# A two-layer Strassen kernel on one core: x of two tiles gets a second home and later splits, and ScalarE copies one PSUM partial sum in more phases

## The reference

```python
x = attention(q, k, v, mem_k, mem_v)              # 3072 x 512
h = x @ moe_w_in                                  # 512 -> 2048
g = np.where(h > 0.0, h, np.exp(np.minimum(h, 0.0)) - 1.0)
x = g @ moe_w_out                                 # 2048 -> 512
r = np.maximum(x @ moe2_w_in, 0.0)
out = (s * (r * r) + b) @ moe2_w_out
```

## Time and profile before

| what | value |
|---|---|
| median of 3 runs | 1153.65 us (1152.37 to 1153.94) |
| profiled execution: its own time | 1152.69 us |
| its span, first to last instruction | 1151.0 us |
| busy share: PE, DVE, ACT, POOL | 96%, 73%, 67%, 34% |
| mean share of the 16 DMA engines' time on the main queue | 84.9% |

### The profile page before, as it was taken

One profiled execution on the slowest core, in us unless ns is written; L12 is line 12 of the kernel. 1 busy time (PEld: TensorE's weight loads), 2 busy tenths in 40 slices (PEclk: granted clock), 3 DMA queues, 4 the chain that ended last, 5 costly groups with the idle time before them and its releaser, 6 DMA issues.

```text
span 1151.0 us, 18156 instructions
## 1 busy us (share of the span) xinstructions
PE 1100.9 (96%) x5787; PEld 876.8 (76%) x5787; DVE 843.8 (73%) x1258; ACT 767.7 (67%) x1806; POOL 392.1 (34%) x427
## 2 busy tenths in 40 slices
PE   7989988989899999989999999999999999999998
PEld 4767666767677777768788787887888888888886
DVE  4895787368957956896887968868848569576485
ACT  4886786577657757756758667667666366674564
POOL 5788789751231432234276113653000000000000
PEclk8998999989999999999999999999999999999999
DMA  9998999999799889859899789998697666776664
GB/s 210 258 272 260 348 321 354 347 286 327 212 269 249 259 244 272 274 184 329 306 357 343 242 260 376 298 351 273 194 275 233 189 198 186 216 220 190 195 189 158
DMA packets 204055, 302.81 MB, mean 263 GB/s; under 512 B 112824, under 2 KB 121016, under 8 KB 203960
## 3 DMA queue, kind: packets, MB, share of 16 engines
q1 hardware_dynamic: 203960, 301.65, 84.9%
HBM read 226.10 MB, written 75.50 MB: 262 GB/s over the span
## 4 chain that ended last, share of the span: by engine, by line
PE 68%; DMA 7%; ACT 6%; POOL 6%; DVE 5%; issue 4%; SPq 4%; ACTq 0%; POOLq 0%; DVEq 0%
PE ps L1003 33%; PE ps L988 30%; DMA w_scratch<-w_new 4%; POOL w_new L786 2%; ACT ps L1083 2%; DMA w_ring<-w_scratch 1%; POOL att L786 1%; ACT elu L1169 1%; PE ps L900 1%; DVE g_lo L1464 1%; SPq L592 1%; PE ps L925 1%; ACT elu L1174 1%; PE ps L952 1%; DVE X L1381 1%
## 5 line engine op out<-in xcount | busy, mean ns | idle before, releaser
L988 PE MATMUL ps<-xc_hi,w_ring 128*128 128x512 f32 x1344 | 435.4, 397 | 6.1 <-DVE X L1433 3.1
L1003 PE MATMUL ps<-g_hi,w_ring 128*128 128x512 f32 x1344 | 421.7, 395 | 15.9 <-issue 7.6
L1003 PEld LDWEIGHTS ps<-g_hi,w_ring 128*128 128x128 f32 x1344 | 249.6, 189 | 75.4 <-issue 14.9
L988 PEld LDWEIGHTS ps<-xc_hi,w_ring 128*128 128x128 f32 x1344 | 253.9, 189 | 64.1 <-issue 3.2
L988 PE MATMUL ps<-xc_lo,w_ring 128*128 128x512 f32 x672 | 263.2, 392 | 0.0
L1003 PE MATMUL ps<-g_lo,w_ring 128*128 128x512 f32 x672 | 263.2, 392 | 0.0
L786 POOL TENSOR_TENSOR w_new<-w_raw,w_new 128x256 fp32r<-128x256 f32 x179 | 165.8, 932 | 226.7 <-ACT w_new L1222 223.8
L1464 DVE TENSOR_TENSOR g_lo<-X,g_hi 128x512 fp32r<-128x512 f32 x240 | 176.9, 741 | 26.1 <-ACT g_hi L1208 25.4
L1208 ACT ACTIVATE g_hi<-X 128x512 fp32r<-128x512 f32 x240 | 148.8, 627 | 62.2 <-PE ps L1003 59.8
L1381 DVE TENSOR_TENSOR X<-s,ps 128x512 f32<-128x512 f32 x144 | 96.1, 682 | 104.6 <-ACT s L1145 77.1
L1003 PEld LDWEIGHTS ps<-g_lo,w_ring 128*128 128x128 f32 x672 | 126.9, 189 | 27.0
(11 more groups left out here) (117 smaller groups left out, 1339.2 us busy)
## 6 DMA issues: line engine op xcount, KB each, us to landing
w_ring<-w_scratch SPq DMA_DIRECT2D x336, 512.0 KB, 4.4
w_scratch<-w_new SPq DMA_DIRECT2D x179, 256.0 KB, 5.3
w_scratch<-att SPq DMA_DIRECT2D x45, 256.0 KB, 5.3
w_raw<-in_moe_w_in SPq DMA_DIRECT2D x16, 512.0 KB, 6.2
w_raw<-in_moe_w_out SPq DMA_DIRECT2D x16, 512.0 KB, 6.2
x_scratch<-y SPq DMA_DIRECT2D x12, 512.0 KB, 6.2
att<-x_scratch SPq DMA_DIRECT2D x12, 512.0 KB, 6.3
out<-elu SPq DMA_DIRECT2D x24, 256.0 KB, 4.4
```

Of the source, the lines that this page charges most:

```text
L988: last = nc.tensor.matmul(bank_of(st.pi, st.i), w[:, a, cols], x[:, st.pi, kk, :], start=(st.pi in (P1, P5, P4) and kk == 0 and n == 0), s ...
L1003: last = nc.tensor.matmul(bank_of(st.pi, d), w[:, a, cols], x[:, k % RING, :], start=(st.pi in (P1, P5) + (P4,) * (1 - st.gr) and st.i == ...
```

## The change

One half of x of tiles 1 and 2 keeps its home in `elu`, the other (kk 1) gets the block X11 of X, which is free late in a down phase; the sums for P6 and P4 go to t_more. Both halves are loaded earlier than the first split (88 and 94), the splits stand at 102 to 105 and 110 to 119, and GpSimd makes three sums of each half and then one more of each. ScalarE copies U2 in every phase.

```diff
-SPLIT_AT = ((92, 93, 95, 96, 97, 98, 100), (107, 108, 110, 111, 113, 115, 117))
-LOAD_AT = (88, 102)
+SPLIT_AT = ((P1, 0, 102), (P1, 1, 103), (P2, 0, 104), (P2, 1, 105), (P5, 0, 110), (P5, 1, 111), (P6, 0, 112), (P6, 1, 113),
+            (P7, 0, 114), (P3, 0, 115), (P4, 0, 116), (P7, 1, 117), (P3, 1, 118), (P4, 1, 119))
+LOAD_AT = (88, 94)
...
-        x_raw = elu[:, :, :]
+        x_raw = [elu[:, :, :], X[:, X11, :, :]]
...
+            if t < TPL and pi in (P6, P4):
+                return t_more[:, kk, :]
             if t < TPL:
-                return x_raw[:, RAW_OF[pi], :]
+                return x_raw[kk][:, RAW_OF[pi], :]
...
-                    sp.wait_ge(x_lo_done, x_count(t) + 7 * kk)
-                    to = x_raw
+                    else:
+                        sp.wait_ge(g_lo_done, PHASE * (2 * t - 1) + QUADS * P5 + QUADS)
+                        sp.wait_ge(t_done, sums_done(t - 1, 1, P6, QUADS - 1))
+                    sp.wait_ge(x_lo_done, x_count(t))
+                    to = x_raw[kk]
...
-                nc.gpsimd.tensor_tensor(t1, x12, x11, ALU.subtract).then_inc(x_sums, 1)
...
+            def sums_of_x(t):
+                n = HEAD_SUMS + 8 * (t - 1)
+                for kk in range(2):
...
+                    pool.wait_ge(x_lo_done, x_count(t) + x_index(t, kk, P1) + 1)
+                    nc.gpsimd.tensor_tensor(x11, x12, x11, ALU.subtract).then_inc(x_sums, 1)
+                    pool.wait_ge(x_sums, n + 3 * kk + 1)
+                    nc.gpsimd.tensor_tensor(t2, x22, x11, ALU.subtract).then_inc(x_sums, 1)
+                    nc.gpsimd.tensor_tensor(x12, x22, x12, ALU.subtract).then_inc(x_sums, 1)
+                for kk in range(2):
+                    x21, t2 = x_from(t, kk, P2), x_from(t, kk, P6)
+                    pool.wait_ge(x_lo_done, x_count(t) + x_index(t, kk, P6) + 1)
+                    nc.gpsimd.tensor_tensor(t2, x21, t2, ALU.subtract).then_inc(x_sums, 1)
...
-                    if r % 6 == 5:
-                        pe.wait_ge(y12_u2, 2 * st.t + i + 1)
-                    else:
-                        pe.wait_ge(s2_done, copies_before(r) + i + 1)
+                    pe.wait_ge(s2_done, 2 * r + i + 1)
...
-                    act.wait_ge(x_lo_done, x_count(d.t + 1))
+                    act.wait_ge(x_lo_done, x_relu(d.t))
...
-                        if x == 12 + d and p.gr == 0:
+                        if x == 12 + d:
                             copy_s2(p.round, d, p.start + QUADS * P6 + 3)
...
-                dve.wait_ge(step_done, p.start + QUADS * P6 + 4)
+                dve.wait_ge(s2_done, 2 * p.round + d + 1)
                 dve.wait_ge(c12_done, 2 * (p.round - 3) + d + 1)
-                add(y_at(X12, d), y_at(X12, d), acc_e[d][:, :], y12_u2)
+                add(y_at(X12, d), y_at(X12, d), s2[:, d, :], y12_u2)
```

More of the change, by code:

```diff
@@ L163, in splits_at @@
     return made
-def copies_before(r):
-    return 2 * (r - r // 6)
 ITEMS0 = 8 * 4 * TPL
@@ L230 @@
 HEAD_ORDER = [(c, pi) for c, pi, _ in HEAD_SPLITS]
-SPLIT_AT = ((92, 93, 95, 96, 97, 98, 100), (107, 108, 110, 111, 113, 115, 117))
-LOAD_AT = (88, 102)
+SPLIT_AT = ((P1, 0, 102), (P1, 1, 103), (P2, 0, 104), (P2, 1, 105), (P5, 0, 110), (P5, 1, 111), (P6, 0, 112), (P6, 1, 113),
+            (P7, 0, 114), (P3, 0, 115), (P4, 0, 116), (P7, 1, 117), (P3, 1, 118), (P4, 1, 119))
+SPLITS = [(pi, kk) for pi, kk, _ in SPLIT_AT]
+LOAD_AT = (88, 94)
 SPLIT_LATE = ((P1, 0, 99), (P1, 1, 100)) + tuple((pi, kk, 106 + 2 * i + kk) for i, pi in enumerate((P2, P5, P6, P7, P4, P3))
@@ L260, in x_index @@
 def x_index(t, kk, pi):
-    return LATE.index((pi, kk)) if t >= TPL else 7 * kk + SPLIT_X.index(pi)
+    return (LATE if t >= TPL else SPLITS).index((pi, kk))
 def x_split_at(g):
[L265 to L272, removed]
+    return [(xt, kk, pi) for xt in range(1, TILES) for pi, kk, at in (SPLIT_AT if xt < TPL else SPLIT_LATE)
+            if g == PER_TILE * (xt - 1) + at]
 def out_block_at(g):
@@ L537, in late_sum, with x_relu, x_sum @@
             return 8 * (t - TPL) + 2 * (SUM_T[pi] - 1) + kk + 1
+        def x_relu(t):
+            return x_count(t) + x_index(t, 0, P4) + 1
+        def x_sum(t, kk, pi):
+            first = HEAD_SUMS + 8 * (t - 1)
+            return first + (7 + kk if pi == P4 else 3 * kk + {P5: 1, P6: 2, P7: 3}[pi])
         def sums_done(t, gr, pi, j):
@@ L807, in prepare @@
                     split_w(m, P3)
[L809 to L814, removed]
-                nc.gpsimd.tensor_tensor(t1, x12, x11, ALU.subtract).then_inc(x_sums, 1)
-                pool.wait_ge(x_sums, n + 1)
-                nc.gpsimd.tensor_tensor(x12, x22, x12, ALU.subtract).then_inc(x_sums, 1)
-                pool.wait_ge(x_lo_done, x_count(t) + x_index(t, kk, P3) + 1)
-                pool.wait_ge(x_sums, n + 2)
-                nc.gpsimd.tensor_tensor(t2, x22, t1, ALU.subtract).then_inc(x_sums, 1)
-                pool.wait_ge(x_lo_done, x_count(t) + x_index(t, kk, P2) + 1)
-                pool.wait_ge(x_sums, n + 3)
-                nc.gpsimd.tensor_tensor(t4, x21, t2, ALU.subtract).then_inc(x_sums, 1)
+            def sums_of_x(t):
+                n = HEAD_SUMS + 8 * (t - 1)
+                for kk in range(2):
+                    pool.wait_ge(x_in[kk], 32 * t)
+                    x12, x22 = (x_from(t, kk, pi) for pi in (P7, P3))
+                    x11 = x_from(t, kk, P1)
+                    t2 = x_from(t, kk, P6)
+                    pool.wait_ge(x_lo_done, x_count(t) + x_index(t, kk, P1) + 1)
[7 more added lines that the diff above has]
+                    nc.gpsimd.tensor_tensor(t2, x21, t2, ALU.subtract).then_inc(x_sums, 1)
             def sums_of_head(c):
@@ L847, in _ @@
             prepare(sets_of(PAIR))
-            for kk in range(2):
-                sums_of_x(1, kk)
+            sums_of_x(1)
             for m in range(SETS, SETS + 4):
                 prepare((m,))
-            for kk in range(2):
-                sums_of_x(2, kk)
+            sums_of_x(2)
             for m in range(SETS + 4, 2 * SETS):
```

5 lines of the change are left out of this document (2 added, 3 removed).

## The result

The change makes the kernel faster, by less than forecast. Eight runs of it have a median of 1150.19 us (1148.11 to 1152.94), eight of the kernel before 1153.8 us (1151.96 to 1155.89): a ratio of 0.997, with a 95% interval of 0.9955 to 0.9984. The forecast was 1147.8, 5.9 us under before; measured are 3.6.

A forecast was written before the change was run, and what follows sets the result against it. TensorE was taken to bound the kernel. The terms −7.6 + 3.0 (tile 1) and −4.1 + 2.8 (tile 0) gave −5.9, so 1153.65 became 1147.8 us; the range was 1141.5 to 1152.5, the forecast's own 1145.0 to 1150.5.

The forecast's parts named there:

- The loss removed: Where the next tile's x is prepared, all waits go: 7.6 us in tile 1, 4.1 in tile 0, together 11.7.
- The mechanism of the new waits: Six GpSimd sums hold the shared SBUF port, so a low part costs VectorE 1.65 us for 0.60; TensorE waits.
- +3.0 (tile 1): Last down phase of tile 1: new waits of 1.1 us at step 108 and 1.9 at step 109.
- +2.8 (tile 0): Tile 0: new waits of 1.5 us at step 108 and 1.0 to 1.1 at step 3 of tile 1; 2.7 to 2.8.
- the list: Timetable of VectorE's operations beside six sums, from step 102 in tile 1 and 103 in tile 0, giving each step's lateness.
- the window of 52 us: Expected profile window of tile 0's last down phase after the change; it was 53.19 before.
- Cost nothing, as said: Loads at 88 and 94, splits at 110 to 119 and ScalarE's U2 copies were each taken as 0 us.
- A: The sums cost nothing on TensorE's path, so all 11.7 us stay gained: 1142.0 us; chance 0.15.
- B: All nine low parts from step 104 on wait for the port, 6.4 us more: 1154.2 us; chance 0.12.
- C: The new waits lower the clock again, 1.7 us in each of tiles 0 and 1: 1151.2 us; chance 0.08.
- D: Weight loads collide with x at steps 100 to 104 of tiles 0 and 1, 9.4 us: 1157.2; chance 0.05.

The follow-up runs named there:

- narrow_sums: The changed kernel with GpSimd's sums of x for tiles 1 and 2 cut to 8 of 512 columns; 1143.14 us, 0.991 of before.
- before_narrow: The kernel before with its sums of x cut to 8 of 512 columns; 1146.67 us, 0.9937 of before.
- hold_half: The changed kernel with GpSimd's three sums of the second half of x held until step 111's low part is made; 1147.03 us, 0.9923 of before.
- late_p2: The changed kernel with the splits for P2 at 108 and 109 instead of 104 and 105; 1146.48 us, 0.9929 of before.
- u2_only: The kernel before with only ScalarE's copies of U2 in the last down phases; 1154.39 us, 1.0009 of before.
- x_only: The changed kernel without ScalarE's extra copies of U2; 1150.95 us, 0.9968 of before.
- spread_no_u2: The changed kernel, second-half sums held until step 111's low part, P2's splits behind P6's, without ScalarE's extra U2 copies; 1142.21 us, 0.9917 of before.
- spread: The changed kernel with the second half's sums held until step 111's low part and P2's splits behind P6's; 1143.87 us, 0.9901 of before.

## Why the prediction was right and wrong

**The loss removed: right.** The forecast was 11.7 us at two places; narrow_sums, which has everything of the change but the length of the sums, measures 11.5. The unit of steps 94 to 105 came to 20.70, and steps 96 to 103 of tile 1 have no wait but 0.14. How the 11.7 came about I had described, but not apportioned: 7.6 were the sums already (before_narrow, with the clock), the late load and the low parts of x in the queue the smaller part.

**The mechanism of the new waits: right.** Low parts at 1.74 to 1.78 us beside six sums, adds to y at 0.68, TensorE waiting at steps 108 and 109. narrow_sums shows the sums as the cause, hold_half and late_p2 that it takes the sums and the low parts of P2 together.

**Their size: the term that failed.** "+3.0 (tile 1)" measured 3.9 and "+2.8 (tile 0)" measured 3.7, 7.6 for 5.8; that is 1.8 of the 2.3 us by which the forecast missed; another 0.2 is the loss removed, 11.5 for 11.7, and the rest is within the interval of the ratio (its ends are −5.2 and −1.8 us; the forecast −5.9 lies just outside). In tile 1 the list started too early and ran too fast. Step 102 began at 496.20. GpSimd's first sum started at 498.50, inside the low part for step 106, but the operation behind it ended at 500.81, 4.6 after that start and not 4.25; and the operations of VectorE came every 1.70 us (500.74, 502.45, 504.15), not 1.65. The low part for step 108 was ready at 9.7 instead of 9.2, that for 109 at 13.1 instead of 12.5. Nothing in the queue absorbs such tenths: step 108 lost 1.65 for 1.1, step 109 1.97 for 1.9, step 110 0.12 for 0. I had taken 1.65 from the starts of two sums, while the two operations of VectorE beside them stood 1.68 apart and took 1.77.

**In tile 0 the list left out a customer of VectorE.** Its first sum came at 2.85 us after the start of step 103 (306.56), not 2.35, and step 107, for which it gave no wait, lost 0.28. Step 109 was "in time" in it. But the scores of the next attention unit, which stand ahead of step 109 on TensorE, need VectorE's copy of the transposed k (L1315). That copy started at 314.15 before and at 316.79 after, behind the sums, and TensorE lost 0.84 there. In the timeline of DVE, before and then after:

```profile
314.15 0.69 DVE L1316 COPY att<-ps 128x512 f32<-128x512 f32 x1 [0.58 <-PE ps L873]
```

```profile
316.79 0.68 DVE L1315 COPY att<-ps 128x512 f32<-128x512 f32 x1
```

Step 108 lost 1.95 for 1.5. Step 3 of tile 1 lost 0.62 for 1.0 to 1.1: the waits ahead of it had let VectorE catch up, and the maximum came only 1.2 us later against TensorE, not 1.4. The list's own terms, 1.5 and 1.0 to 1.1, add up to 2.5 to 2.6 and not to the 2.8 of the sum, so the miss in tile 0 is 1.1 to 1.2. And the window of 52 us that I gave for tile 0's last down phase was hit (52.16) by luck: my terms give 53.19 − 4.1 + 1.5 = 50.6.

**Cost nothing, as said:** the loads (weights took 3.4, 4.5 and 9.4 us from issue to landing, for 3.3, 4.4 and 9.0, with no wait for w_ring at steps 100 to 106), the splits at 110 to 119, the copies of U2 (u2_only, x_only, spread_no_u2).

**The rivals.** A needed the sums to cost nothing: they cost 7.6, and the version in which they cost nearly nothing, spread, is another order. B needed nine stretched operations; six were. The measurement went its way, by 1.8 us of its 6.4. Its reason, that GpSimd is slowed in turn, is half right: the sums took up to 1.77 us, but the row held no more than six of VectorE's operations. C fell: waits of 1.49 and 1.70 us in tile 1 and of 1.76 in tile 0 left the clock at 1.00. D fell with the loads.
